# Scaling queries and keys one chunk ahead on VectorE, in the attention part of an attention and mixture-of-experts kernel

## The reference

```
mag = sqrt(a_re**2 + a_im**2); a = (a_re + i*a_im) * min(mag, 0.999) / (mag + 1e-6)
for t in range(768):
    S = a[t][:, None] * S + outer(k[t], v[t])        # complex S, real k and v
    y[t] = q[t] @ real(S)
```

## Time and profile before

| | us |
|---|---|
| median of 3 runs (977.53 to 978.83) | 978.09 |
| the profiled execution, its own time | 978.09 |
| its span, first to last instruction | 976.3 |
| attention, start to about | 290 |

### The profile page before, as it was taken

How to read it: one execution, slowest core, us unless ns; L and a number is a source line. 1 busy time by engine, 2 the same in 40 slices (tenths; PEclk the granted TensorE clock), 3 DMA queues, 4 the chain that set the end, 5 groups by cost and what they waited for, 6 DMA issues and landing times.

```text
span 976.3 us, 18188 instructions
## 1 busy us (share of the span) xinstructions
PE 940.3 (96%) x5904; PEld 836.7 (86%) x5905; DVE 438.7 (45%) x794; ACT 441.9 (45%) x742; POOL 510.1 (52%) x429
## 2 busy tenths in 40 slices
PE   5999999999879999999999999999999999999997
PEld 4777878887877989989999898999998999999997
DVE  5898898898846333433433432222222122222111
ACT  7999888997711222222222333333333333333322
POOL 4134656656464986767759923343243433423433
PEclk9999999999989999999999999999999999999999
DMA  3642363340153645335355520010010000000000
GB/s 121 205 139 83 113 238 99 101 137 2 64 183 94 205 133 167 113 105 169 113 169 169 130 57 17 9 41 17 9 49 17 29 21 17 33 1 1 33 1 32
DMA packets 74123, 83.89 MB, mean 86 GB/s; under 512 B 57653, under 2 KB 63305, under 8 KB 71497
## 3 DMA queue, kind: packets, MB, share of 16 engines
q1 hardware_dynamic: 67048, 47.20, 17.5%
q0 software_dynamic: 6144, 34.65, 10.2%
q10 hardware_dynamic: 864, 1.19, 0.3%
HBM read 65.59 MB, written 17.38 MB: 85 GB/s over the span
## 4 chain that ended last, share of the span: by engine, by line
PE 77%; ACT 10%; DVE 5%; issue 5%; DMA 1%; POOL 1%; ACTq 1%; SPq 0%; POOLq 0%; DVEq 0%
PE bank L2168 21%; PE bank L2181 20%; PE bank L2156 12%; PE bank L2131 12%; PE bank L2141 3%; PE bank L1098 2%; DVE neglog L850 1%; PE bank L1180 1%; PE bank L1138 1%; PE bank L1166 1%; PE bank L1140 1%; PE bank L1108 1%; PE bank L1121 1%; DVE neglog L857 1%; ACT log_sq L643 1%
## 5 line engine op out<-in xcount | busy, mean ns | idle before, releaser
L1922 POOL TENSOR_TENSOR act_r<-act_f,act_r 128x512 fp32r<-128x512 f32 x96 | 124.7, 1298 | 258.2 <-ACT act_r L1984 258.1
L2181 PE MATMUL bank<-w_out_r,act_r 128*128 128x384 f32 x1152 | 216.6, 336 | 0.3 <-POOL act_r L1922 0.3
L2168 PE MATMUL bank<-x,w_in_r 128*128 128x512 f32 x864 | 215.7, 394 | 0.0
L2181 PEld LDWEIGHTS bank<-w_out_r,act_r 128*128 128x128 f32 x1152 | 203.8, 188 | 9.1 <-POOL act_r L1922 0.6
L2063 DVE TENSOR_TENSOR act_f<-bank,small 128x512 f32<-128x512 f32 x96 | 66.5, 692 | 286.9 <-ACT small L1981 286.9
L2168 PEld LDWEIGHTS bank<-x,w_in_r 128*128 128x128 f32 x864 | 160.6, 187 | 30.1
L1981 ACT ACTIVATE small<-bank 128x512 f32<-128x512 f32 x96 | 57.5, 599 | 194.7 <-PE bank L2168 194.5
L2131 PE MATMUL bank<-wm,x_tr 128*128 (+1 forms) x522 | 129.1, 401 | 1.5 <-issue 1.0
L2156 PE MATMUL bank<-wm,h_tr 128*128 (+1 forms) x696 | 125.6, 336 | 0.0
L2156 PEld LDWEIGHTS bank<-wm,h_tr 128*128 128x128 f32 x696 | 121.5, 188 | 2.5
L2131 PEld LDWEIGHTS bank<-wm,x_tr 128*128 128x128 f32 x522 | 96.0, 188 | 23.3 <-issue 2.2
(11 more groups left out here) (195 smaller groups left out, 1363.9 us busy)
## 6 DMA issues: line engine op xcount, KB each, us to landing
stage<-moe_w POOLq DMA_DIRECT2D x12, 1536.0 KB, 7.3
qkv_in<-in_qkv SPq DMA_DIRECT2D x24, 576.0 KB, 6.0
a_in<-in_a SPq DMA_DIRECT2D x11, 768.0 KB, 5.2
stage<-moe_w SPq DMA_DIRECT2D x4, 1536.0 KB, 7.1
x_q<-x_sorted SPq DMA_DIRECT2D x116, 48.0 KB, 1.9
y_sorted<-y_b SPq DMA_DIRECT2D x29, 192.0 KB, 1.9
xg<-y_sorted SPq DMA_DIRECT2D x96, 48.0 KB, 1.9
stage<-w_out POOLq DMA_DIRECT2D x2, 1536.0 KB, 7.0
```

What stands on the lines that cost most here:

```text
L1922: pool.tensor_tensor(a[:, 1, :], act_f[f % 2][:, :], a[:, 0, :].bitcast(F32), ALU.subtract).then_inc(s_gl, 1)
L2168: last = pe.matmul(h_bank[f % 2][:, :], w_in_r[:, wp, t * F2 + f * P:t * F2 + (f + 1) * P], window_part(w, xp)[:, t, :], start=(t == 0 and ...
L2181: last = pe.matmul(o_bank[j][:, 0:W], a[:, ap, j * P:(j + 1) * P], w_out_r[:, wp, f * W:(f + 1) * W], start=(f == 0 and n == 0), stop=(f = ...
```

## The change

In even chunks from 2 on, and in odd chunks from 3 on, `scale(n + 1)` is no longer done ahead of `rotate(n + 1)`. Instead `scale(n + 2)` is done late in chunk n: in an even chunk behind the phases and ahead of `pick_experts`, in an odd chunk as the last thing. In chunk 1 both `scale(2)` and `scale(3)` are done, in chunk 0 nothing moves. In odd chunks `numerator` and the phases change places.

```
@@ -1050,7 +1050,8 @@
                 turns(chain_angle(n))
             if n % B == 2 and B < n < NCH - 2:
                 positions(n // B - 1)
-            scale(n + 1)
+            if n < 2:
+                scale(n + 1)
             if n % 2 == 0:
                 rotate(n + 1)
                 mask(n, 1)
@@ -1059,6 +1060,8 @@
                     half_tangent(u)
                 for m in summed(n):
                     phases(m)
+                if n > 0:
+                    scale(n + 2)
                 if n % B == 0 and 0 < n < NCH:
                     pick_experts(n // B - 1)
                 if n == NCH - 2:
@@ -1070,10 +1073,11 @@
                 if u is not None:
                     left_half(u)
                     sum_squares(u)
+                if u is not None:
+                    numerator(u)
                 for m in summed(n):
                     phases(m)
-                if u is not None:
-                    numerator(u)
+                scale(n + 2)
             if n in (NCH - 3, NCH - 2):
                 first_trailing(n - NCH + 3)
             if n == NCH - 3:
```

## The result

The changed kernel takes 1005.6 us (median of 4 runs, 1003.24 to 1007.92) against 978.5 us before; the ratio is 1.0279, with a 95% interval of 1.0263 to 1.0296. It is slower, as forecast, but by 27 us and not by 10: the time lies above the range.

What follows compares the result with a forecast made beforehand. The prediction took the cycle from one `decay_log` through TensorE, ScalarE, `cosine_log` and `cap` to the next as the bound. It summed 978.1 + 13.4 - 2.5 - 1.3 = 987.7 us, own range 985.5 to 992.8, wider range 979.5 to 995.5.

Steps and rivals of the forecast that it cites:

- The cycle: Steady attention: `decay_log`, TensorE, ScalarE, `cosine_log`, `cap`, `decay_log` follow without slack; 20.89 us for chunks 10 and 11.
- Part 1: Odd chunks: `scale` leaves the way to `rotate`, 0.95 us sooner; gain 0, cost taken as 0 (2 us if uncovered).
- Part 2: Odd chunks: freed `carry_in` lets `cosine_log` start sooner in chunks 6, 8, 10, 14, 18; 0.5 us each, gain 2.5.
- Part 3: Even chunks 2 to 18: freed `sine_eps` delays `decay_log` by 1.49 us, nine times; cost 13.4 us.
- both borders: End of `cosine_log`: `cap` goes before `sine_eps`; end of `cap`: `sine_eps` goes before `decay_log`.
- the list of signs: What the profile after would show, among it `decay_log` growing from 0.96 to about 2.3 us.
- Everything behind `decay_log` (...) shifts along: `sum_logs`, `fall` and `rise` and ScalarE's next stretch move by the delay, as the cycle has no slack.
- the case that the pause might give something back: The prediction would be wrong if TensorE's pause gave something back in the odd chunk; no size given.
- Part 4: Last chunks: TensorE waits for VectorE there, which comes sooner; about 1.3 us gained, bounds 0 and 1.4.
- the two waits named in the prediction: TensorE's waits ahead of chunk 20's transposes (0.4 us gained) and ahead of the logits (0.95 us gained).
- VectorE keeping its place at border 2: Behind `cap`, `decay_log` runs before `sine_eps` in all nine pairs; only gains stay, 974.3 us; chance 0.13.
- GpSimd keeping its place at border 1: Behind `cosine_log`, `sine_eps` runs before `cap`; 2.3 us a pair, 21 us, 995.3 us; chance 0.05.

Runs made afterwards that it cites:

- the guard: The changed kernel with one wait more: GpSimd starts `sine_eps` of chunks 2 to 18 only when `decay_log` of the same unit is done; 974.8 us.
- e11_pick_first: The changed kernel with the guard, and `pick_experts` ahead of `scale(n + 2)` in chunks divisible by four; 974.5 us.
- e9_carry_free: The kernel before with one count changed: `carry_in` waits for the `scale` of one chunk earlier, VectorE's order untouched; 982.1 us.
- e3_fill: The changed kernel with 14 transposes of zeros on TensorE ahead of `sum_logs` in chunks 2 to 18, filling the pause; 987.7 us.
- e10_guard_no_tail: The changed kernel with the guard, and the `scale` of chunks 20 to 23 in its old place; 976.0 us.
- e2_before_free: The kernel before, with `sine_eps` of chunks 2 to 18 waiting for the `scale` of one chunk earlier, VectorE's order untouched; 1013.3 us.
- e5_one_pair: The changed kernel with the guard in all chunks but chunk 10, so that one collision is left; 978.8 us.
- e8_before_pause: The kernel before, with three memsets on VectorE between `cap` and `decay_log` in chunks 2 to 18, GpSimd untouched; 1015.5 us.
- e4_halves: The changed kernel with `sine_eps` of chunks 2 to 18 as two GpSimd instructions of 128x384 instead of one of 128x768; 990.2 us.
- e6_guard_late_carry: The changed kernel with the guard, and `carry_in` held back until the first half of `rotate` on VectorE is done; 986.1 us.

## Why the prediction was wrong, by its own steps

- **The cycle** (`decay_log`, TensorE, ScalarE, `cosine_log`, `cap`) and its rule that `cap` ends 0.42 behind GpSimd: right in all nine chunks of the changed kernel.
- **Part 1, scale itself**: right. With the guard the moved `scale` costs nothing that shows (3.9 us gained between medians, where parts 2 and 4 give 4.2), and e11_pick_first shows that its overrun in every fourth chunk costs nothing.
- **Part 2, carry_in**: the size was right, 2.9 us against 2.5 (the nine starts of `decay_log`, with the guard and before), and `cosine_log` comes earlier in the five chunks that were named. That it comes with a condition was not seen: the prediction gave it to the earlier start alone, and e9_carry_free shows that without the moved `scale` the earlier start is a loss of 4.5 us, the clock's part in it included.
- **Part 3, both borders and the price**: right. L857 grew to 2.44 us ("about 2.3 us" in the list of signs did not fit the prediction's own 2.91 behind `cosine_log`, which makes 2.45), 1.49 us for a pair was forecast, and e3_fill, in which the clock is kept up, shows 1.49; 12.9 us lie between its time and the guard's, where the sum had 13.4. The Trainium skill's rule ("SBUF — State Buffer", section "SBUF: two separate sides") that the second one is blocked until the first has ended holds here, with 0.81 us behind it for `decay_log` and not the whole 0.96.
- **The step that failed** stands behind it: "Everything behind `decay_log` (...) shifts along". That took TensorE's pace for given. A delay of 1.49 us, which leaves TensorE pauses of 1.5 to 1.9 us, was put at its length; in its place the runs show its length and a fall of the granted clock to 0.50 for 3.4 us, or 10.2. That term was missing. It is 17.9 us between the medians of the changed kernel and e3_fill, 14.9 us of it between the first and the last `decay_log` of the profiled executions. The prediction named the case that the pause might give something back; it took. Without it the sum was 987.7 us, and e3_fill, where it is absent between 60 and 260 us, measures 987.7. That both agree to the last digit is luck: its four executions lie from 986.46 to 988.48, and falls of the clock behind 260 us are in it too.
- **Part 4, the last chunks**: 1.3 us forecast, 1.3 us in the profiles of the guard and of e10_guard_no_tail. The size is shown; that it comes from the two waits named in the prediction is not, since with the guard TensorE has other waits there (1.63 us ahead of the scores at 259.36, which the kernel before has not).
- **The rivals**: VectorE keeping its place at border 2 was seen in no chunk of these runs. GpSimd keeping its place at border 1 was seen once, in e2_before_free.

Open: what decides whether the clock falls, and for how long. It stays down for 10.2 us behind the first pause of the changed kernel, the one of e5_one_pair, the last of e2_before_free and three of e8_before_pause, and for 3.4 us behind most others. It does not follow from the length of the pause: e4_halves has falls behind pauses of 0.72 us and none behind four of 1.10, and in the kernel before TensorE pauses 1.54 us at 259.70 and 1.48 at 273.98 with the clock at 1.00 until 282 us. Also open is what decided border 1 in chunk 8 of e2_before_free. Not tried: a guard placed elsewhere, or the signed numerator's place alone.

## What to carry to other kernels

A wait that looks idle can be what keeps two engines off a shared port: before it goes, look at what its owner will run against, and guard by the event that matters (here `decay_log`) instead of by a neighbour that happens to come late enough. Where TensorE is kept at full clock by a stream with short gaps only, price a new pause with the clock's fall beside its length; here that more than doubled the loss, and filling the pause with idle transposes took that part away. With the right guard the same change is 0.36% faster than the kernel before.

## What the runs showed of the hardware that was not expected

- In a stream that is 96% busy over the span, pauses of TensorE of 1.5 to 3.2 us ahead of `sum_logs` came with a fall of the granted clock from 2.4 to 1.2 GHz each time, during the pause or at most 1.0 us behind it: 28 of 28, in the changed kernel, e2_before_free, e8_before_pause and e5_one_pair. Transposes of zeros in the pause kept it at 1.00 in nine of nine (e3_fill).
- Shorter pauses there had it at times, and not the longer of them more often: 1.1 us in three of nine (e4_halves, e6_guard_late_carry), 0.72 us in three of four (e4_halves), 0.43 us once in each of three executions of guarded kernels and never in the two others. Pauses of 1.5 us in the last chunks of the kernel before had none.
- Small GpSimd instructions were slower where they ran beside VectorE's `numerator` and `scale` (e6_guard_late_carry): four of 8 columns took 2.06 us instead of 1.04. And a GpSimd instruction on one partition of 384 columns holds a VectorE instruction on 128 partitions with two SBUF inputs for 0.8 us (e9_carry_free).
- At the border between two GpSimd instructions a waiting `cap` went first in all nine chunks of the changed kernel, but in one chunk of another it waited through three of them.
